# A fused attention and two-MLP kernel in float32: order of the chunks, sources and slots in the last product

## The chip, the cores and the metric

One core of a Trainium2 chip. The metric is the device time of one execution in microseconds (us), as the median of several runs. The engines are named as in the profile: PE (TensorE, matmuls), PEld (its weight loads), DVE (VectorE), ACT (ScalarE), POOL (GpSimd), SP (SyncE, which issues nearly all DMAs; "SPq" is its queue).

## The reference

Windowed attention over 4 batches of 8 heads, 576 positions, head size 64; then two MLPs over the 2304 tokens. Everything is float32.

```python
def _attn_ref(q, k, v):
    scores = scale * np.matmul(q, k.transpose(0, 1, 3, 2))
    mask = (rel >= 0) & (rel < 64)
    scores = np.where(mask, scores, -1000000000.0)
    ...                                  # softmax
    return np.matmul(attn, v)
def _moe_ref(x, w1, w2, w3, w_out):      # (2304,512) -> (2304,512)
    a = x @ w1
    b = x @ w2
    h = a * b @ w3
    return h @ w_out
def _moe2_ref(x, w_in, w_out):           # 512 -> 2048 -> 512
    h = x @ w_in
    g = np.maximum(0.01 * h, h)
    return g @ w_out
```

## The kernel before

**Splitting.** Each float32 operand of a large product is split into a high part (ACT, a Copy into float32r) and a low part (DVE, operand minus high part). A product is then three matmuls: high by high, high by low, low by high (`three_passes`, L367 to L369).

**Seven products.** Each large product is one level of a Strassen-like scheme: 7 products P1, P5, P6, P2, P7, P3, P4 (in this order) of half-size blocks. They share banks: P1, P6, P7 and P4 use one pair of banks (alpha), P5 and P3 another (gamma), P2 a third (beta). So copies and sums stand between them: ACT copies P1, P5 and P6 out (`copy_p1` L817, `copy_p5` L827, `copy_u2` L835), DVE adds P2, P7, P3 to these (`make_c11` L1237, `make_c22` L1247, `make_c12` L1257). In `bank_waits` P6 waits for the copy of P1, P7 for the copy of P6 (u2), P3 for the copy of P5, P4 for c22. Weight sums are made once (for w_out in rounds 2 to 9 by `out_sums`, stored in DRAM as `weight_sums`).

**Stages.** (1) w3 times moe w_out, 16 slots of pieces, beside the first attention steps. (2) 12 rounds of a and b and their product P, stored in DRAM as `p_between`. (3) The y product, 3 chunks of 768 tokens; 42 parts of P (`load_ty`, `split_ty` L848 and L1305) and then 7 blocks of x2. (4) The first product of the second MLP, 12 rounds r = HR0 to OR0 - 1, h = 0 to 11: four rounds for each of three chunks, a round making two of 16 row blocks of g for one chunk. Its 7 blocks of g (leaky ReLU on ACT L873 and L881, sums on DVE L1344, L1348, L1353) lie in `g_st` and are stored by SP as 7 DMAs of 384 KB into `g_between` (`store_g`, L570). (5) The second product: 84 parts k, in the order `T_SEQ` of (chunk, product, jp), jp = 0 to 3. A part is 2 x 768 columns of g from 384 KB: SP loads it (`load_t`, L587) into one of 8 slots `t_raw`, ACT and DVE split it (`split_t`, L897 and L1358) into block k modulo 7, PE does 12 matmuls of 384 columns on it (`second_product`). tk is part k's load.

**The slots.** `t_raw` 0 and 1 are spare places; 2 to 7 lie over `g_st` and can be used only when all of g is stored. So the first eight parts (`TEARLY`), all of chunk 0, go through slots 0 and 1 in turn; a load waits for the split of the part before it in its slot.

**The weights of the second product.** The 8 units of w_out (F_OUT to F_OUT + 7, here F0 to F7) take the place of the 8 units of w_in in the last four rounds (8 to 11), two per round: unit n is free when P4 has used it. SP loads a unit (L453 384 KB, L461 512 KB) into one of two places `unit_raw` when the split of the unit two before it is done; ACT (L767) and DVE (L1106) split it in two pieces each.

**Order.** All engines run lists written out in Python loops, in order; nothing is scheduled. An engine that waits holds everything behind it. In the old rounds 9 to 11 ACT does: copies of P1, split of the first late unit, copies of P5, (round 11: split t0), copies of u2, split of the second late unit, then the leaky steps.

## Time and profile before

| | us |
|---|---|
| median of 3 runs (all: 766.12, 770.91, 770.90) | 770.9 |
| the profiled execution | 769.24 |
| its span (first to last instruction) | 767.2 |
| PE busy | 747.2 |
| DVE busy | 531.9 |
| ACT busy | 420.6 |
| mean granted clock of PE | 0.991 |

The span is the time that the rows below cover; 2.0 us of the execution lie around it. "Granted clock" is the share of PE's full 2.4 GHz; a stretch at 0.50 is at 1.2 GHz. Times in rows are us from the start of the span. A matmul's row is longer than the step from one to the next, since they overlap.

### The profile page before, as it was taken

To read this page: it belongs to the slowest core of one execution; us is meant where nothing else is said; L and a number is where in the kernel's file an instruction comes from. 1 tells how busy PE (TensorE), PEld (TensorE's weight loads), DVE (VectorE), ACT (ScalarE), POOL (GpSimd) and SP (SyncE) were. 2 spreads that over 40 slices of the span, in tenths; PEclk is the share of its full clock that TensorE was granted. 3 is DMA by queue.
4 is the path that set the end of the run, shared out by engine and by line. 5 is a ranking of instruction groups with operands and counts; after the bars stand their busy time and mean duration, and the time that the engine had idled before them with its cause. 6 is when DMAs were issued, how large, how long until landed. Compare 5 with 4: busy or idle time off the path is not lost.

```text
span 767.2 us, 13105 instructions
## 1 busy us (share of the span) xinstructions
PE 747.2 (97%) x4744; PEld 720.9 (94%) x4744; DVE 531.9 (69%) x836; ACT 420.6 (55%) x901; POOL 95.3 (12%) x122
## 2 busy tenths in 40 slices
PE   8999999999999999999999999999897899999998
PEld 6787999999999999999999999999897799999998
DVE  4977998788656868698777968567786555455442
ACT  4866577546564344566646665454764544544441
POOL 1533374503243000000000000000000000000000
PEclk9999999999999999999999999999999899999999
DMA  9885777656873389889858888997997977778731
GB/s 327 283 288 165 233 231 235 216 156 214 283 226 129 127 268 343 298 247 331 296 192 296 305 304 304 327 306 246 400 370 241 385 209 238 211 205 231 218 108 62
DMA packets 100576, 192.89 MB, mean 251 GB/s; under 512 B 8224, under 2 KB 58272, under 8 KB 100512
## 3 DMA queue, kind: packets, MB, share of 16 engines
q1 hardware_dynamic: 94208, 179.08, 71.0%
q10 hardware_dynamic: 6304, 12.98, 4.4%
q8 instruction: 38, 0.62, 0.3%
q14 instruction: 26, 0.21, 0.1%
HBM read 120.06 MB, written 71.96 MB: 250 GB/s over the span
## 4 chain that ended last, share of the span: by engine, by line
PE 75%; DMA 9%; DVE 7%; ACT 3%; issue 3%; SPq 2%; POOL 1%; DVEq 0%; ACTq 0%
PE acc L367 13%; PE acc L369 13%; PE acc L368 13%; PE ps_scores L1565 3%; PE ps_more L367 3%; PE ps_more L369 3%; PE ps_more L368 3%; PE ps_values L1549 2%; PE ps_values L367 2%; PE ps_values L368 2%; PE ps_values L369 2%; PE ps_turned L1557 2%; PE ps_scores L367 2%; DMA p_between<-arena 2%; PE ps_scores L368 2%
## 5 line engine op out<-in xcount | busy, mean ns | idle before, releaser
L1358 DVE TENSOR_TENSOR parts<-arena,parts 128x768 fp32r<-128x768 f32 x72 | 68.5, 958 | 67.6 <-ACT parts L897 67.6
L367 PE MATMUL acc<-parts,weights_a 128*128 128x384 f32 (+1 forms) x300 | 105.8, 353 | 1.3 <-DVE arena L1295 0.7
L369 PE MATMUL acc<-parts,weights_a 128*128 128x384 f32 (+1 forms) x300 | 103.2, 344 | 0.0
L368 PE MATMUL acc<-parts,weights_a 128*128 128x384 f32 (+1 forms) x300 | 103.1, 344 | 0.0
L897 ACT ACTIVATE parts<-arena 128x768 fp32r<-128x768 f32 x72 | 60.6, 847 | 72.7 <-PE acc L369 35.0
L367 PE MATMUL acc<-parts,weights_b 128*128 128x384 f32 x296 | 99.9, 337 | 0.0
L369 PE MATMUL acc<-parts,weights_b 128*128 128x384 f32 x296 | 98.9, 334 | 0.0
L368 PE MATMUL acc<-parts,weights_b 128*128 128x384 f32 x296 | 98.9, 334 | 0.0
L778 ACT ACTIVATE arena<-arena,negmax 128x128 f32<-128x128 f32 x144 | 56.0, 391 | 28.4 <-DVE negmax L1144 28.4
L367 PEld LDWEIGHTS acc<-parts,weights_a 128*128 128x128 f32 x300 | 56.6, 189 | 5.3 <-DVE parts L1171 1.0
L369 PEld LDWEIGHTS acc<-parts,weights_a 128*128 128x128 f32 x300 | 56.5, 188 | 2.0
L368 PEld LDWEIGHTS acc<-parts,weights_a 128*128 128x128 f32 x300 | 56.7, 189 | 1.5
L873 ACT ACTIVATE arena<-arena 128x384 f32<-128x384 f32 x72 | 35.9, 525 | 40.5 <-DVE arena L1237 18.6
L367 PEld LDWEIGHTS acc<-parts,weights_b 128*128 128x128 f32 x296 | 55.6, 188 | 0.1
L368 PEld LDWEIGHTS acc<-parts,weights_b 128*128 128x128 f32 x296 | 55.6, 188 | 0.0
L369 PEld LDWEIGHTS acc<-parts,weights_b 128*128 128x128 f32 x296 | 55.6, 188 | 0.0
L848 ACT ACTIVATE parts<-arena 128x768 fp32r<-128x768 f32 x42 | 35.4, 848 | 33.7 <-PE ps_turned L369 10.7
L707 POOL TENSOR_TENSOR arena<-arena,rsum 128x512 f32<-128x512 f32 x36 | 37.5, 1042 | 126.1 <-DVE rsum L1152 126.1
L1305 DVE TENSOR_TENSOR parts<-arena,parts 128x768 fp32r<-128x768 f32 x42 | 39.6, 954 | 14.7 <-ACT parts L848 14.6
L1565 PE MATMUL ps_scores<-arena 128*128 128x128 f32 x288 | 38.1, 275 | 0.1
L1565 PEld LDWEIGHTS ps_scores<-arena 128*128 128x128 f32 x288 | 35.3, 192 | 0.6 <-issue 0.4
L1139 DVE SCALAR_TENSOR_TENSOR arena<-ps_scores,arena 128x512 f32<-128x512 f32 x36 | 24.6, 685 | 11.9 <-PE ps_scores L1565 11.5
(230 smaller groups left out, 1887.8 us busy)
## 6 DMA issues: line engine op xcount, KB each, us to landing
g_between<-arena SPq DMA_DIRECT2D x84, 384.0 KB, 4.8
arena<-g_between SPq DMA_DIRECT2D x84, 384.0 KB, 3.9
arena<-qk_steps SPq DMA_DIRECT2D x36, 512.0 KB, 4.2
arena<-p_between SPq DMA_DIRECT2D x42, 384.0 KB, 5.6
arena<-v_steps SPq DMA_DIRECT2D x36, 256.0 KB, 3.2
p_between<-arena SPq DMA_DIRECT2D x24, 384.0 KB, 5.2
x_between<-arena ACTq DMA_DIRECT2D x21, 384.0 KB, 5.2
arena<-x_between SPq DMA_DIRECT2D x21, 384.0 KB, 5.3
```

Of the source, the lines that this page charges most:

```text
L367: eng.matmul(out_ap, w_hi, m_hi, start=start, stop=False, skip_group_check=resumed)
L368: eng.matmul(out_ap, w_hi, m_lo, start=False, stop=False, skip_group_check=resumed)
L369: return eng.matmul(out_ap, w_lo, m_hi, start=False, stop=stop, skip_group_check=resumed)
L707: pool.tensor_tensor(probs[:, r], probs[:, r], rsum[:, r * HP:(r + 1) * HP].unsqueeze(2).to_broadcast([P, HP, KW]), ALU.mult).then_inc(pro ...
L778: act.activation(probs[:, r, u], probs[:, r, u], ACT.Exp, bias=negmax[:, r * HP + u:r * HP + u + 1], scale=1.0, accum_out=sums[:, r * HP + ...
L848: act.activation(block_places[k % NPROD][:, 0:BW], ty_raw[TY_SLOT[k]], ACT.Copy).then_inc(ty_hi, 1)
L873: act.activation(g, g, ACT.Prelu, alpha=SLOPE).then_inc(g_done[q], 1)
L897: act.activation(block_places[k % NPROD][:, 0:BW], t_raw[T_SLOT[k]], ACT.Copy).then_inc(t_hi, 1)
L1139: dve.scalar_tensor_tensor(out=probs[:, r], in0=ps_s[:, :].rearrange("p (h k) -> p h k", h=HP), scalar=float(D) ** -0.5, in1=picked.unsque ...
L1305: dve.tensor_tensor(b[:, BW:2 * BW], ty_raw[TY_SLOT[k]], b[:, 0:BW].bitcast(F32), ALU.subtract).then_inc(ty_lo, 1)
L1358: dve.tensor_tensor(b[:, BW:2 * BW], t_raw[T_SLOT[k]], b[:, 0:BW].bitcast(F32), ALU.subtract).then_inc(t_lo, 1)
L1565: last = pe.matmul(ps_s[:, w], qk[:, g % 2, w], qk[:, g % 2, DM + u * P:DM + (u + 1) * P], start=True, stop=True)
```

## The change

1. **Chunk order** `O_CHUNK = (2, 0, 1)`: the second product starts with the chunk made last. Its parts jp = 0 to 2 come from DRAM (rounds 8 to 10), its seven parts jp = 3 (round 11) are split from `g_st` itself (`T_HELD`, `t_source`, `t_ready`). Round 11 stores nothing, and 7 loads are left out. Inside products P6 to P4 of that chunk the held part comes first.
2. **Slots** are given out by `t_slots`: the place that was free first, slots 2 to 7 once the held blocks under them are split and the last sums are made.
3. **SP**: t0 and t1 are issued after round 10's last stores, not before its fills; t2 and t3 before F7; t4 and on after F7.
4. **Round 9**: F0 is split behind the copies of u2 (ACT) and c11 (DVE), F1 behind the leaky step of c22 (ACT) and c12 (DVE). Round 11's end: t3, F6, t4, F7.
5. **Parts of P**: 12 and 13 are issued in the last a and b round; 14 and 15 ahead of two fills.
6. **Start**: the mask and the pieces of slot 2 are loaded earlier, v(0), the first fill and v(1) later.

```diff
-TY_LOAD = {(9, 6): (0, 1), (10, 3): (2, 3), (10, 8): (4, 5), (11, 2): (6, 7), (11, 5): (8, 9)}
+TYEARLY = 10
+TY_LOAD = {..., (11, 5): (8, 9), (11, 9): (TYEARLY + 2,), (11, 11): (TYEARLY + 3,)}
...
-T_SLOT = [k % SPARE if k < TEARLY else (k - TEARLY + SPARE) % TRAW for k in range(TB)]
...
+O_CHUNK = (NC2 - 1, *range(NC2 - 1))
 T_SEQ = [(0, i, jp) for i, jp in ((0, 0), (0, 1), (0, 2), (1, 0), (1, 1), (1, 2), (0, 3), (1, 3))]
-T_SEQ += [(c, i, jp) for c in range(NC2) for i in range(NPROD) for jp in range(JP) if c > 0 or i > 1]
+T_SEQ += [(0, i, jp) for i in range(2, NPROD) for jp in (3, 0, 1, 2)]
+T_SEQ += [(c, i, jp) for c in range(1, NC2) for i in range(NPROD) for jp in range(JP)]
+T_HELD = [c == 0 and jp == JP - 1 for c, _, jp in T_SEQ]
+def t_slots():
+    freed = [-1, -1] + [1 + max(T_SEQ.index((0, i, JP - 1)) for i in pair) for pair in ((0, 1), (0, 1), (P6, P2), (P6, P2), (P7, P3), (P7, P3))]
+    ...
+        best = min(range(TRAW), key=lambda n: freed[n])
...
+        def t_source(k):
+            if T_HELD[k]:
+                return g_st[:, :, G_AT[T_SEQ[k][1]]]
+            return t_raw[T_SLOT[k]].rearrange("p (j t) -> p j t", j=2)
...
             def load_t(k):
-                c, i, jp = T_SEQ[k]
+                q, i, jp = T_SEQ[k]
+                if T_HELD[k]:
+                    return
+                c = O_CHUNK[q]
...
+                if T_SLOT[k] >= SPARE and T_USES[k] == 1:
+                    sp.wait_ge(gt2_made, 2 * HR)
+                    sp.wait_ge(gt4_made, 2 * HR)
+                if T_AFTER[k] > 0:
+                    sp.wait_ge(t_lo, T_AFTER[k])
...
+            sp.dma_start(mask_s[:, :], masks).then_inc(mask_in, 16)
             load_qk(1)
-            sp.dma_start(mask_s[:, :], masks).then_inc(mask_in, 16)
+            for i in pieces_for(2):
+                load_piece(i)
             load_v(0)
+            load_fill(0)
             load_v(1)
-            load_fill(0)
...
-                if h == HR - 2:
-                    for k in range(SPARE):
-                        load_t(k)
+                if h == HR - 1:
+                    load_t(0)
+                    load_t(1)
+                    load_fill(late)
+                    load_t(2)
+                    load_t(3)
+                    load_fill(late + 1)
+                    continue
...
-                if h > HR - ROUNDS:
+                if h > HR - ROUNDS + 1:
                     split_fill(late, 0)
                     split_fill(late, 1)
...
                 for s in range(2):
                     copy_u2(r, s)
...
+                if h == HR - ROUNDS + 1:
+                    split_fill(late, 0)
+                    split_fill(late, 1)
```

ScalarE in round 9, before: the copies of P1 (L817, banks ps_scores and ps_turned), the split of F0 (L767 into weights_a), the copies of P5 (L827) and of u2 (L835), the split of F1.

```order
L817 ACTIVATE arena<-ps_scores 128x384
L817 ACTIVATE arena<-ps_turned 128x384
L767 ACTIVATE weights_a<-arena 128x768
L767 ACTIVATE weights_a<-arena 128x1024
L827 ACTIVATE arena<-ps_values 128x384
L827 ACTIVATE arena<-ps_more 128x384
L835 ACTIVATE arena<-ps_scores 128x384
L835 ACTIVATE arena<-ps_turned 128x384
L767 ACTIVATE weights_a<-arena 128x768
L767 ACTIVATE weights_a<-arena 128x1024
L873 ACTIVATE arena<-arena 128x384 x6
```

The same place after (L860, L870, L878 are the copies, L810 the split of a unit, L916 the leaky step):

```order
L860 ACTIVATE arena<-ps_scores 128x384
L860 ACTIVATE arena<-ps_turned 128x384
L870 ACTIVATE arena<-ps_values 128x384
L870 ACTIVATE arena<-ps_more 128x384
L878 ACTIVATE arena<-ps_scores 128x384
L878 ACTIVATE arena<-ps_turned 128x384
L810 ACTIVATE weights_a<-arena 128x768
L810 ACTIVATE weights_a<-arena 128x1024
L916 ACTIVATE arena<-arena 128x384 x4
L810 ACTIVATE weights_a<-arena 128x768
L810 ACTIVATE weights_a<-arena 128x1024
```

F0's split has moved behind the copies of u2, F1's behind four of the six leaky steps.

SyncE's queue from the stores of round 9 to those of round 10, before: L570 stores g, L587 loads a part of g, L453 and L461 load a late unit.

```order
L570 DMA g_between<-arena 128x2x384 x6
L587 DMA arena<-g_between 128x768 x2
L453 DMA arena<-w_out_units 128x768
L461 DMA arena<-weight_sums 128x1024
L570 DMA g_between<-arena 128x2x384
L453 DMA arena<-w_out_units 128x768
L461 DMA arena<-weight_sums 128x1024
L570 DMA g_between<-arena 128x2x384 x6
```

After (L611 stores, L628 loads a part, L494 and L502 load a unit), on to the end of round 11:

```order
L611 DMA g_between<-arena 128x2x384 x6
L494 DMA arena<-w_out_units 128x768
L502 DMA arena<-weight_sums 128x1024
L611 DMA g_between<-arena 128x2x384
L494 DMA arena<-w_out_units 128x768
L502 DMA arena<-weight_sums 128x1024
L611 DMA g_between<-arena 128x2x384 x6
L628 DMA arena<-g_between 128x768 x2
L494 DMA arena<-w_out_units 128x768
L502 DMA arena<-weight_sums 128x1024
L628 DMA arena<-g_between 128x768 x2
```

The two loads of g that stood ahead of F4 now stand behind the six last stores of round 10; round 11's stores are gone.

ScalarE from the copies of P5 to those of u2 in round 11, after (L940 is the split of t0; before, the same rows with L827, L897 and L835):

```order
L870 ACTIVATE arena<-ps_values 128x384
L870 ACTIVATE arena<-ps_more 128x384
L940 ACTIVATE parts<-arena 128x768
L878 ACTIVATE arena<-ps_scores 128x384
L878 ACTIVATE arena<-ps_turned 128x384
```

Here nothing moved: the split of t0 keeps its place.

## Rows read from the trace of the kernel before

**Rows 1.** page: busy us by engine, and groups splitting g (busy, mean ns)
```profile
PE 747.2 (97%) x4744; PEld 720.9 (94%) x4744; DVE 531.9 (69%) x836; ACT 420.6 (55%) x901; POOL 95.3 (12%) x122
...
L1358 DVE TENSOR_TENSOR parts<-arena,parts 128x768 fp32r<-128x768 f32 x72 | 68.5, 958 | 67.6 <-ACT parts L897 67.6
...
L897 ACT ACTIVATE parts<-arena 128x768 fp32r<-128x768 f32 x72 | 60.6, 847 | 72.7 <-PE acc L369 35.0
```

**Rows 2.** waits of PE: total us, times, longest us
```profile
PE ps_values L367 <- DVE parts L1358: 4.1, 1, 4.1
PE acc L367 <- DVE weights_a L1358: 3.7, 1, 3.7
PE ps_scores L367 <- ACT arena L835: 3.5, 2, 2.2
```

**Rows 3.** timeline of PE: start, duration, instruction, [idle before <-releaser]
```profile
537.40 0.34 PE L369 MATMUL acc<-parts,weights_a 128*128 128x384 f32 x1
...
539.96 0.69 PE L367 MATMUL ps_scores<-parts,weights_a 128*128 128x384 f32 x1 [2.22 <-ACT arena L835]
...
543.22 0.33 PE L368 MATMUL ps_turned<-parts,weights_a 128*128 128x384 f32 x1
...
570.61 0.33 PE L367 MATMUL ps_scores<-parts,weights_b 128*128 128x384 f32 x1
...
582.92 0.34 PE L369 MATMUL acc<-parts,weights_b 128*128 128x384 f32 x1
...
599.17 0.69 PE L367 MATMUL acc<-weights_a,weights_b 128*128 128x384 f32 x1 [3.75 <-DVE weights_a L1358]
...
604.66 0.34 PE L369 MATMUL ps_more<-parts,weights_b 128*128 128x384 f32 x1
```

**Rows 4.** timeline of ACT, rounds 9 and 11
```profile
536.98 1.79 ACT L767 ACTIVATE weights_a<-arena 128x768 fp32r<-128x768 f32 x2 [4.96 <-DMA arena<-weight_sums]
...
539.42 0.49 ACT L835 ACTIVATE arena<-ps_scores 128x384 f32<-128x384 f32 x1
...
567.38 0.86 ACT L897 ACTIVATE parts<-arena 128x768 fp32r<-128x768 f32 x1
```

**Rows 5.** timelines of ACT and PE, start of the kernel
```profile
13.68 0.63 ACT L755 ACTIVATE parts<-arena 128x512 fp32r<-128x512 f32 x1 [4.39 <-DMA arena<-w_tiles]
...
15.77 0.50 PE L367 MATMUL acc<-parts 128*128 128x512 f32 x1 [1.79 <-DVE parts L1094]
```

**Rows 6.** timelines of ACT and PE, y product of chunk 0
```profile
324.00 0.85 ACT L848 ACTIVATE parts<-arena 128x768 fp32r<-128x768 f32 x1 [3.85 <-DMA arena<-p_between]
...
326.31 0.41 PE L367 MATMUL ps_scores<-parts,weights_b 128*128 128x384 f32 x1 [1.27 <-ACT arena L835]
```

**Rows 7.** stretch: us, busy by engine (PE first), PEclk, DMA share, GB/s
```profile
540.00:572.00 32.00, 32.00 (x177) 32.00 (x178) 26.14 (x41) 23.42 (x43) 0.00 (x0) 0.95 1.05 395
```

**Rows 8.** load of F2's second half (L461), issue and landing
```profile
L461 SPq DMA_DIRECT2D arena<-weight_sums x1: 760/760/760, 542.8 to 542.8; - x1
...
DMA to landing us min/median/max: 6.7/6.7/6.7
```

**Rows 9.** timelines of DVE and SP at the end of round 10
```profile
563.80 1.02 DVE L1353 TENSOR_TENSOR arena<-arena 128x384 f32<-128x384 f32 x2
...
568.03 0.75 SPq L453 DMA_DIRECT2D arena<-w_out_units  x1
```

**Rows 10.** landing of the load issued at 568.03 (L453)
```profile
DMA to landing us min/median/max: 5.5/5.5/5.5
```

**Rows 11.** landing of t0, issued at 553.55 (L587)
```profile
DMA to landing us min/median/max: 6.2/6.2/6.2
```

**Rows 12.** load t3 (L587), issue and landing
```profile
L587 SPq DMA_DIRECT2D arena<-g_between x1: 320/320/320, 575.2 to 575.2; - x1
...
DMA to landing us min/median/max: 3.7/3.7/3.7
```

**Rows 13.** landing of round 8's last two g stores (L570), 535 to 543
```profile
DMA to landing us min/median/max: 9.9/10.3/10.6
```

More of the change, by code:

```diff
@@ L153 @@
 TRAWY = 6
-TYEARLY = 10
 HRING = 4
@@ L182 @@
 T_SEQ = [(0, i, jp) for i, jp in ((0, 0), (0, 1), (0, 2), (1, 0), (1, 1), (1, 2), (0, 3), (1, 3))]
-T_SEQ += [(c, i, jp) for c in range(NC2) for i in range(NPROD) for jp in range(JP) if c > 0 or i > 1]
-T_USED = [sum(jp < JP - 1 for _, _, jp in T_SEQ[:k + 1]) for k in range(TB)]
+T_SEQ += [(0, i, jp) for i in range(2, NPROD) for jp in (3, 0, 1, 2)]
+T_SEQ += [(c, i, jp) for c in range(1, NC2) for i in range(NPROD) for jp in range(JP)]
+T_STEP = [sum(e[:2] == T_SEQ[k][:2] for e in T_SEQ[:k]) for k in range(TB)]
+T_USED = [sum(step < JP - 1 for step in T_STEP[:k + 1]) for k in range(TB)]
+T_HELD = [c == 0 and jp == JP - 1 for c, _, jp in T_SEQ]
+def t_slots():
+    freed = [-1, -1] + [1 + max(T_SEQ.index((0, i, JP - 1)) for i in pair) for pair in ((0, 1), (0, 1), (P6, P2), (P6, P2), (P7, P3), (P7, P3))]
+    uses, slot, after, count = [0] * TRAW, [], [], []
+    for k in range(TB):
+        best = min(range(TRAW), key=lambda n: freed[n])
+        if T_HELD[k]:
+            best = None
+        slot.append(best)
+        after.append(None if best is None else freed[best])
+        if best is not None:
+            uses[best] += 1
+            freed[best] = k + 1
+        count.append(None if best is None else uses[best])
+    return slot, after, count
+T_SLOT, T_AFTER, T_USES = t_slots()
 def build(nc, qk_steps, v_steps, masks, w3, wo, w12, w_in, w_out, out):
@@ L643, in _ @@
             load_ty(TYEARLY + 1)
+            load_ty(TYEARLY + 4)
+            load_ty(TYEARLY + 5)
             load_fill(F_IN + 2)
-            load_ty(TYEARLY + 2)
             load_fill(F_IN + 3)
-            for k in range(TYEARLY + 3, NTY):
+            for k in range(TYEARLY + 6, NTY):
                 load_ty(k)
@@ L1039, in _ @@
                 leaky(r, 2, c22_done)
+                if h == HR - ROUNDS + 1:
+                    split_fill(late + 1, 0)
+                    split_fill(late + 1, 1)
                 if last:
@@ L1050, in _ @@
                     leaky_c21(r, s)
-                    if h == HR - 1:
-                        split_fill(NFILL - 2 + s, 0)
-                        split_fill(NFILL - 2 + s, 1)
                 if last:
                     split_hx(NPROD * c + P7)
-            split_t(3)
-            for k in range(TROUND, TB + NPROD):
+            for n in range(2):
+                split_t(3 + n)
+                for part in range(2):
+                    split_fill(NFILL - 2 + n, part)
+            for k in range(TROUND + 1, TB + NPROD):
                 if k < TB:
@@ L1497, in _ @@
                     make_c12(r, s)
+                if h == HR - ROUNDS + 1:
+                    split_fill(late + 1, 0)
+                    split_fill(late + 1, 1)
                 if last:
@@ L1520, in _ @@
                     split_hx(NPROD * c + P7)
-            for k in range(TROUND, TB + NPROD):
+            for k in range(TROUND + 1, TB + NPROD):
                 if k < TB:
```

98 lines of the change are left out of this document (52 added, 46 removed).

## The prediction

> **What bounds the kernel now.** I read the busy shares, then what TensorE waits for, then the timelines around those waits, then the DMA landings. TensorE is busy 747.2 of 767.2 us [rows 1], so the change can win only where it idles or runs at half clock. Its waits are few [rows 2]: 4.1 and 3.7 us for splits of g (DVE L1358), 2.2 and 1.3 us for the copies of u2 (ACT L835). A matmul of 384 columns comes every 0.1734 us (71 steps from 570.61 to 582.92 [rows 3]), so 12 take 2.08 us and the 84 of a round 14.56.
>
> *Round 9.* Between the matmuls at 537.40 and 543.22 lie 11 steps, which should take 1.91 us and took 5.82 [rows 3]: 3.9 us lost, 2.4 of them the wait and 1.5 the half clock (1.2 GHz) that followed it. ScalarE stood 4.96 us before the split of the late weight unit F0 (F0 to F7: the units of w_out), whose DMA landed at 536.9, and the copies of p5 and u2 stood behind it [rows 4].
>
> *Into the second product.* From 582.92 to 604.66 there are 54 steps: 9.36 us of work in 21.74, 12.4 lost, and 0.1 more in the following steps: 12.5 us. Two waits and two stretches at half clock make them up; after the second, 17 steps took 5.49 us instead of 2.95, so 2.5 us went to the clock [rows 3].
>
> *Start and y product.* A wait of 1.79 us at 15.77 ends with a piece whose DMA ScalarE had awaited for 4.39 us, until 13.68 [rows 5]. A wait of 1.27 us at 326.31 has the same form: part 12 of P came from DRAM 3.85 us late and the copy of u2 stood behind it [rows 6]. Everything else is about 1.5 us of crumbs and is left alone.
>
> **Part 1, start.** Pieces 4 and 5 are issued before both loads of v, and before the two of the first fill. That is 1.0 MB less ahead of them, 2.6 us at the 395 GB/s of a full queue [rows 7]. The piece that came at 13.68 comes near 11, and the 1.8 us wait goes. Mask and qk change places at no cost: nothing waited for qk. VectorE paces this stretch in places, so I bound the gain by 0 and 2.1 us (the wait and a later 0.3) and take 1.8.
>
> **Part 2, parts 12 and 13 of P.** They are issued in the last round of a and b, behind parts 8 and 9, so they are there long before 320. Their slots need only splits 0 and 1. Gain 1.27 us and 0.24 of the slow first matmul (0.41 against 0.17): 1.5, at least 0.
>
> **Part 3, round 9.** F0 is split behind the copies of u2, F1 behind the leaky steps of c22. The copies then need no DMA, and product P7 starts at 537.57: 3.9 us back. But what comes next hangs on the DMA queue. It is full from 540 to 572 (share 1.05, 395 GB/s) [rows 7], so data lands when it did, while TensorE is 3.9 us earlier. F2 still lands at 542.8 + 6.7 = 549.5 [rows 8]; behind it ScalarE has its split, two copies of p5 and the first copy of u2, 2.9 us from start to end in round 9 (536.98 to 539.91 [rows 4]). So P7 of round 10 starts at 552.5, where it could at 552.1 (four products, 8.3 us, after 543.8): 0.4 us given back (0 to 2.5, the upper end with the half clock of rows 3). Net 3.5 us. The next neighbour, c22 of round 10 behind VectorE's split of F3, I find about 0.2 us ahead of P4; a miss there lies inside the same 2.5.
>
> **Part 4, the last chunk first.** Seven g stores and seven loads of g (2.7 MB each way) go. The first loads, t0 and t1, change place: before, SP issued t0 at 553.55, ahead of round 10's fills, and now behind the last store of round 10. Nothing is moved on ScalarE here: split t0 (L897) stays between the copies of p5 and of u2 of round 11 [rows 4]. So t0 is now a condition of P7 in round 11, which began at 570.61 [rows 3].
>
> When does t0 land? In the old trace round 10's last sum ended at 564.82 and the DMA behind the stores was issued at 568.03 [rows 9], 3.2 us later, and landed 5.5 us after that, at 573.5 [rows 10]. Now t0 stands in that place. Round 10's sums are some 2.5 us earlier (3.5 us, less 1 for DVE's wait for F3), which gives 565.5 for its issue. Two 384 KB loads less ahead of it give 2.0 us: 571.5. The other way, 565.5 plus 5.5 or 6.2 (the old t0 landed 6.2 after issue, also behind a burst of stores [rows 11]) gives 571.0 to 571.7. I take 571.5. Split 0.85 and the first copy of u2 0.5, with gaps, open P7 at 572.9. TensorE would be there at 570.6 - 3.5 = 567.1: a new wait of 5.8 us. The half clock behind it cost 1.5 to 2.5 us in rows 3; I take 2.0. Bounds: t0 lands 3.7 us after issue, as a load in a quiet queue did [rows 12], then P7 opens at 570.6 and this costs 3.5 + 1.5 = 5.0; or it lands 8 us after issue, then 7.8 + 2.5 = 10.3.
>
> From P7 on, first P7 to P4 (6.24 us) and 2.0: the second product starts at 572.9 + 8.2 = 581.1. Then the splits (0.85 on ScalarE, 0.96 on VectorE [rows 1]):
> - P7 at half clock ends near 576.8, its sums c22 at 577.5; behind them VectorE ends t1 at 578.3, and behind c12 t2 at 580.4.
> - t3's slot is free at 578.3; landed 3.7 later, 582.1; split on VectorE behind the g sums, 584.2. Part 3 is due at 587.3.
> - F6 and t4 are done at 587.2, part 4 is due at 589.4. F6 and F7 no longer queue with g stores.
> - t5 waits for t3's split, lands at 588.0 and is split behind F7 and the last g sums at 591.2; due at 591.5. This margin of 0.3 us is the thinnest.
> - parts 6, 7 and 8 come from where g lies, need no DMA, and let t9, t10, t11 run ahead.
>
> So the old 12.5 us go and 7.8 come: 4.7 us net (bounds 12.5 - 5.0 = 7.5, and 12.5 - 10.3 - 3 for waits at part 5 = -0.8). Later parts cost the same matmuls; chunks 0 and 1 were stored long before, and the last chunk's end is the same code.
>
> **Sum.** 1.8 + 1.5 + 3.5 + 4.7 = 11.5 us off the profiled execution's 769.24: 757.7. The runs' median is 770.9, their lowest 766.1, so the profiled one is 1.7 below the median and 3.1 above the lowest; between these I say 758.5.
>
> **Rivals.**
> - *t0 hides.* If the queue drains in round 10, or the splits arrive so that the copies of u2 run ahead of t0, the 7.8 us don't come: 751. For it: seven stores less, but those are round 11's, too late; against it: the queue's share of 1.05 and the order on ScalarE. Chance 0.13.
> - *t0 passes the stores.* It lands 3.7 us after issue, as in a quiet queue, and its wait costs 5.0 instead of 7.8: 755.7. The landings of 5.5 and 6.2 behind such bursts speak against it [rows 10, 11]. Chance 0.08. The Trainium skill, "DMA: Bandwidth & Descriptors", section "Queues, rings and completion order", would allow it: completion is not first in, first out per issuing engine, and a later DMA may finish its write before an earlier one.
> - *Splits too late at parts 3 to 5.* A landing 1.5 us longer than 3.7 adds 3 us at part 5 and another 1.5 of half clock: 763, and with a start that gains nothing, 765. Chance 0.17.
> - *The two-slot chain decides, slower.* t2 to t5 use only slots 0 and 1; t3 waits for t1's split and t5 for t3's. Every us of landing over 3.7 counts twice. With 10.6 us, the longest of the g stores of round 8 [rows 13], that is 13.8 - 0.3 + 2.5 = 16 us: 774. It passes the old time from landings of 8.1 us on. For it: such landings exist; against: they were seen in a full queue, and here only F7 is beside. Chance 0.05.
> - *The change does less than it says.* The held parts wait for the last leaky step and sums, and if DVE's new order (t3, F6, t4, F7, then the last sums) makes these late, the slots 2 and 3 open late and parts 11 on wait: 766. The held parts have 5 us of slack, so 0.05.
> - The forecast has 0.52, with its own range 755 to 763.
>
> A difference of 1%, 7.7 us, is about what a measurement tells from no change; the border is 763.2. The forecast and the first two rivals lie below it almost whole, the third half across, the fifth within 1%: faster 0.76, same 0.19, slower 0.05. The range reaches from the first rival to the third and fifth: 750 to 767.
>
> **What would show it.** Right: no wait for ACT L835's counterpart in round 9; a wait of about 5.8 us before P7 of round 11, released by the copy of u2, ScalarE idle before split t0 for a DMA out of g_between, and half clock behind it; no wait over 1 us in the second product; 1.8 and 1.3 us waits gone at the start and in the y product. Wrong: if P7 of round 11 doesn't wait, the queue was not the limit I take it for, and the time is near 751; if waits stand before parts 3 to 5, the landings in the new order are longer than 3.7 us; if the 1.8 us come back before 100 us, VectorE paces the start.

## The result, and the profile after

| | before | after |
|---|---|---|
| median, 4 runs of each on one chip (us) | 770.65 (766.12 to 770.91) | 760.14 (758.99 to 761.03) |
| profiled execution, its span | 769.24, 767.2 | 761.03, 759.2 |
| mean granted clock of PE | 0.991 | 0.996 |

The ratio is 0.9882, with a 95% interval of 0.9845 to 0.9919: about 9 us, or 6 to 12. The two medians lie 10.5 us apart, but one of the four runs of before is 4 us below the other three. Predicted were 758.5 us and 750 to 767. The time was right; the gain was less than the forecast's. Of its four terms one gave nothing that the times show, and another about 0.6 us on average.

Line numbers have moved: the copies of P1, p5 and u2 are now L860, L870 and L878, the split of a part is L940 (ACT) and L1410 (DVE), a load of g is L628, a store of g L611. The page's header and busy shares first, beside [rows 1]:

```profile
span 759.2 us, 13176 instructions
PE 743.8 (98%) x4744; PEld 717.4 (94%) x4744; DVE 530.9 (70%) x836; ACT 420.6 (55%) x901; POOL 96.1 (13%) x122
```

TensorE has the same 4744 matmuls and is busy 3.4 us less, mostly half clock that is gone; the other 4.6 of the 8.0 us of span are waiting. What TensorE waited for over the span (total, times, longest), beside [rows 2]:

```profile
PE ps_scores L387 <- ACT arena L878: 6.0, 1, 6.0
PE acc L387 <- DVE parts L1410: 1.5, 1, 1.5
PE ps_more L1791 <- POOL ident L744: 1.5, 1, 1.5
PE acc L387 <- DVE parts L1145: 1.2, 2, 0.9
PE acc L387 <- ACT arena L878: 0.6, 1, 0.6
```

The waits of 4.1, 3.7, 2.2 and 1.3 us are gone, and one of 6.0 and one of 1.5 (P6) stand in their place. The row of POOL is the wait for the first data of the kernel, at 1.52 us in both traces. The timeline of TensorE has three waits from round 10 on, beside [rows 3]:

```profile
549.73 0.44 PE L387 MATMUL acc<-parts,weights_b 128*128 128x384 f32 x1 [0.61 <-ACT arena L878]
...
570.74 0.69 PE L387 MATMUL ps_scores<-parts,weights_b 128*128 128x384 f32 x1 [5.99 <-ACT arena L878]
...
597.92 0.41 PE L387 MATMUL acc<-parts,weights_b 128*128 128x384 f32 x1 [1.49 <-DVE parts L1410]
```

They are P7 of round 10, P7 of round 11, and the first matmul of P6 in the second product (part 8). ScalarE at the second and third of these places, beside [rows 4]:

```profile
561.49 0.48 ACT L870 ACTIVATE arena<-ps_more 128x384 f32<-128x384 f32 x1
569.46 0.84 ACT L940 ACTIVATE parts<-arena 128x768 fp32r<-128x768 f32 x1 [7.49 <-DMA arena<-g_between]
570.21 0.47 ACT L878 ACTIVATE arena<-ps_scores 128x384 f32<-128x384 f32 x1
...
592.79 0.85 ACT L940 ACTIVATE parts<-arena 128x768 fp32r<-128x768 f32 x1 [2.54 <-DMA arena<-g_between]
595.09 1.58 ACT L940 ACTIVATE parts<-arena 128x768 fp32r<-128x768 f32 x2 [1.45 <-DMA arena<-g_between]
596.58 0.82 ACT L940 ACTIVATE weights_a<-arena 128x768 fp32r<-128x768 f32 x1
597.31 0.85 ACT L860 ACTIVATE arena<-acc 128x384 f32<-128x384 f32 x2
```

The first three rows are the predicted wait as it was predicted: ScalarE stands 7.5 us before the split of t0, the copy of u2 is behind it, and TensorE starts P7 0.06 us after the end of that copy. In the last four, the copy of P1 stands behind the splits of parts 10 to 13, and P6 needs the bank that this copy empties; the experiments take that up, since the profile names VectorE for this wait. The landing of t0, issued at 563.09 behind round 10's last stores, beside [rows 11]:

```profile
DMA to landing us min/median/max: 6.3/6.3/6.3
```

And the stretches (busy by engine with PE first, granted clock, DMA share, GB/s), beside [rows 7]:

```profile
560.00:565.00 5.00, 4.75 (x28) 4.43 (x26) 2.24 (x3) 1.97 (x4) 0.00 (x0) 1.00 1.05 387
565.00:570.00 5.00, 0.00 (x0) 0.00 (x0) 0.00 (x0) 0.54 (x1) 0.00 (x0) 0.94 0.99 333
570.00:575.00 5.00, 4.26 (x13) 4.26 (x14) 4.37 (x7) 4.57 (x9) 0.00 (x0) 0.50 0.44 151
575.00:580.00 5.00, 5.00 (x27) 5.00 (x27) 4.22 (x6) 3.15 (x7) 0.00 (x0) 0.87 0.51 153
```

In such a row the first figure is the length of the stretch, the next five are the busy times, and the seventh is the granted clock. TensorE runs 13 matmuls in the third stretch, where full clock has room for 25: half clock (1.2 GHz) from 570.7 to 576.3, 17 steps in 5.58 us where 2.95 would do, so 2.6 us behind a wait of 6.0.

At the start and in the y product, beside [rows 5, 6], the row of 1.79 us is gone, a smaller one has come 5 us earlier, and ScalarE has no wait for a DMA near 324:

```profile
10.69 0.50 PE L387 MATMUL acc<-parts,weights_a 128*128 128x512 f32 x1 [0.90 <-DVE parts L1145]
```

### The profile page after: what moved, and what is told of

It reads as the page before. It is cut to its first block, busy times and chain, and to the rows that moved or that the text cites. A ratio compares the mean times of both kernels' runs of the same rounds, so it can differ in the third digit from the quotient of the medians.

```text
span 759.2 us, 13176 instructions
## 1 busy us (share of the span) xinstructions
PE 743.8 (98%) x4744; PEld 717.4 (94%) x4744; DVE 530.9 (70%) x836; ACT 420.6 (55%) x901; POOL 96.1 (13%) x122
## 4 chain that ended last, share of the span: by engine, by line
PE 75%; DMA 9%; DVE 7%; issue 3%; ACT 3%; SPq 2%; POOL 1%; DVEq 0%; ACTq 0%
PE acc L387 13%; PE acc L389 13%; PE acc L388 13%; PE ps_scores L1623 3%; PE ps_more L387 3%; PE ps_more L389 3%; PE ps_more L388 3%; DMA g_between<-arena 3%; PE ps_values L1607 2%; PE ps_turned L1615 2%; PE ps_values L387 2%; PE ps_values L388 2%; PE ps_values L389 2%; PE ps_scores L387 2%; PE ps_turned L389 2%
## 5 line engine op out<-in xcount | busy, mean ns | idle before, releaser
L1410 DVE TENSOR_TENSOR parts<-arena,parts 128x768 fp32r<-128x768 f32 x72 | 68.7, 957 | 71.7 <-ACT parts L940 71.7
L940 ACT ACTIVATE parts<-arena 128x768 fp32r<-128x768 f32 x72 | 60.7, 847 | 77.9 <-PE acc L389 35.0
L916 ACT ACTIVATE arena<-arena 128x384 f32<-128x384 f32 x72 | 35.8, 525 | 40.3 <-DVE arena L1288 18.5
```

The costliest lines, as they stand in the source:

```text
L916: act.activation(g, g, ACT.Prelu, alpha=SLOPE).then_inc(g_done[q], 1)
L940: act.activation(block_places[k % NPROD][:, 0:BW].rearrange("p (j t) -> p j t", j=2), t_source(k), ACT.Copy).then_inc(t_hi, 1)
L1410: dve.tensor_tensor(lo, t_source(k), hi.bitcast(F32), ALU.subtract).then_inc(t_lo, 1)
```

## Three intervals that all runs are read by

TensorE's instructions are the same in every kernel here, so the same matmul can be found in each trace, and the time between two of them compared. Three intervals, from the starts of the rows of TensorE's timeline: (s) the start of the 49th matmul of 512 columns, which tells what the start has cost so far; (y) from the 1,009th to the 1,401st matmul of 384 columns, the first part of the y product; (z) from the 2,251st to the 3,501st, which is from round 8 nearly to the end. Without waits and at full clock, z would be 1250 x 0.1734 = 216.8 us.

| kernel | s | y | z | ratio to before, 95% |
|---|---|---|---|---|
| before | 25.38 | 69.46 | 233.33 | |
| before_round9 | 25.89 | 67.95 | 232.06 | 0.9995 [0.9985, 1.0006] |
| after | 23.39 | 67.95 | 228.52 | 0.9882 [0.9845, 0.9919] |
| after_again | 22.45 | 67.95 | 228.01 | 0.9897 [0.9877, 0.9916] |
| after_round9_back | 23.30 | 67.95 | 227.54 | 0.9897 [0.9877, 0.9916] |
| after_y_back | 23.09 | 68.14 | 227.39 | 0.9886 [0.9868, 0.9904] |
| after_start_back | 24.90 | 67.94 | 228.71 | 0.9936 [0.9914, 0.9958] |
| order_alone | 26.22 | 68.70 | 228.23 | 0.9931 [0.9915, 0.9947] |
| split_behind_u2 | 23.18 | 67.95 | 225.33 | 0.9871 [0.9853, 0.9888] |
| t0_in_round10 | 22.71 | 67.95 | 225.96 | 0.9876 [0.9858, 0.9895] |
| copy_p1_early | 22.71 | 67.95 | 226.19 | 0.9860 [0.9841, 0.9879] |
| t0_r10_copy_early | 22.70 | 67.95 | 223.29 | 0.9824 [0.9808, 0.9840] |
| sums_later | 22.99 | 67.94 | 220.18 | 0.9788 [0.9772, 0.9804] |
| sums_later_round9_back | 22.66 | 67.94 | 219.53 | 0.9783 [0.9765, 0.9801] |

From the 2,651st to the 3,501st matmul all of them take 147.33 or 147.34 us. Whatever the kernels differ by in z happens before it.

The ratios are against runs of the kernel before on the same chip. The intervals of the ratios are 0.8 to 2.8 us to either side, so differences between two kernels of under 2 us are read from z as much as from the time.

## Experiments

**after_again**: the changed kernel once more, as the measure for the three others of its group.

> The changed kernel once more, as the measure for the three kernels beside it. Both theories: 760 us, within 1 us of its four runs (758.99 to 761.03), with a wait of 6 us before P7 of round 11.

Measured: 759.45 us (757.76 to 760.74), before beside it 767.4. The wait before P7 of round 11 is 5.2 us in this trace. The gain is 7.9 us by this ratio, 9.1 by the first; the kernel before had medians of 767.4, 768.1 and 768.7 us in the three later groups of runs (13, 9 and 11), not the 770.9 of its first three.

**before_round9**: the new order of round 9 alone, put into the kernel before. The three places below in ScalarE's list are behind the copies of P1, of u2, and behind the leaky step of c22; VectorE's list changes in the same way.

```diff
-                if h > HR - ROUNDS:
+                if h > HR - ROUNDS + 1:
                     split_fill(late, 0)
                     split_fill(late, 1)
 ...
-                if h > HR - ROUNDS:
+                if h == HR - ROUNDS + 1:
+                    split_fill(late, 0)
+                    split_fill(late, 1)
+                if h > HR - ROUNDS + 1:
                     split_fill(late + 1, 0)
                     split_fill(late + 1, 1)
 ...
                 leaky(r, 2, c22_done)
+                if h == HR - ROUNDS + 1:
+                    split_fill(late + 1, 0)
+                    split_fill(late + 1, 1)
```

> The kernel before with one part of the change alone: in round 9 F0 is split behind the copies of u2 and F1 behind the leaky step of c22 (ACT) and c12 (DVE). Theory A (the stall of 3.9 us goes, and the full DMA queue takes some back, since F2 lands when it did): no wait before P7 of round 9, one of 0.4 to 0.8 us before P7 of round 10, and from round 11 on the loads in slots 0 and 1, which hang on the queue and on splits, keep the waits of 4.1 and 3.7 us or lengthen them a little: 767 us at the profile, 2 to 3 us less than the kernel before beside it. Theory B (all 3.9 us are kept): 3.9 us less. Theory C (the queue gives nothing back to TensorE): the waits into the second product grow by the whole 3.9 us: no difference.

Measured: 767.0 us, ratio 0.9995 [0.9985, 1.0006]. By the time it is theory C: nothing. The wait in round 9 is gone and TensorE is ahead at the 2,401st matmul by 3.2 us more than at the 2,251st, as the forecast said. But the waits of TensorE in this trace are

```profile
PE ps_values L367 <- DVE parts L1364: 5.3, 1, 5.3
PE acc L367 <- DVE weights_a L1364: 3.4, 1, 3.4
```

5.3 us where before waited 4.1, for the same part 3. At the 2,601st matmul 1.4 of the 3.2 us are left, and 1.3 in z. So the waits for the splits of g take back more than half in this trace, not all as theory C has it, and the times show nothing of what is left.

**split_behind_u2**: the split of t0 stands behind the copies of u2 and the leaky steps of c11 (ACT), behind c22 (DVE). If the wait of 6.0 us is the order on ScalarE, it goes.

```diff
-                if h == HR - 1:
-                    split_t(0)
                 for s in range(2):
                     copy_u2(r, s)
 ...
                 if h == HR - 1:
+                    split_t(0)
                     split_t(1)
```

The diff shows ScalarE's list; the same is done in VectorE's.

> The changed kernel, with the split of t0 moved behind the copies of u2 and the first leaky step of round 11 on ACT, and behind c22 on DVE; the loads keep their place. Theory A (the split's place in ACT's queue makes the wait of 6.2 us before P7 and the 2.6 us of half clock behind it): no wait before P7 of round 11. The second product could then start near 570.5 instead of 579.6; t0, landed at 569.4, is split at 571.3, and t2 to t5, which go through two slots, hold parts 2 to 5: waits of 1 to 2 us each, part 6 some 3 to 4 us earlier than now. 756 to 757 us. Theory B (the landings set the end whatever the order): the waits before parts 0 to 5 add up to what the wait before P7 was, 760 us.

**t0_in_round10**: t0 and t1 are loaded in round 10, behind its fill F4 and its second store of g, so that they land before ScalarE comes to them.

```diff
                 if h == HR - 1:
-                    load_t(0)
-                    load_t(1)
                     load_fill(late)
 ...
                 if h > HR - ROUNDS:
                     load_fill(late)
+                if h == HR - 2:
+                    load_t(0)
                 store_g(r, 0)
 ...
                 store_g(r, 1)
+                if h == HR - 2:
+                    load_t(1)
```

> The changed kernel, with the load of t0 issued in round 10 right behind F4's, and that of t1 behind round 10's second store of g; all splits keep their place. Theory A (the place of t0 in the DMA queue makes the wait): t0 lands near 561, the wait before P7 of round 11 is under 1 us; t2 lands 2 us later than the stores of round 10, near 573.5, and holds part 2 by some 1.5 us, t4 and t5 hold theirs by as much: 756 us. Theory B (the queue is full, so each transfer only trades places with another): F5 or the stores come 2 us later, and the waits before the second product's parts 2 to 5 give all back: 760 us.

Measured: split_behind_u2 757.59 us, ratio 0.9871 [0.9853, 0.9888]; t0_in_round10 757.84 us, ratio 0.9876 [0.9858, 0.9895]. These intervals overlap with those of the changed kernel, so what follows is read from z. In both the wait of 6.0 us and the half clock behind it, 8.6 us together, are gone; from the 2,251st to the 2,501st matmul TensorE is 8 to 9 us faster. Yet z is shorter by only 2.1 to 3.2 us. That is more than theory B's nothing and under theory A's 3 to 4 us. The rest has gone into waits that did not exist. TensorE in t0_in_round10:

```profile
578.82 0.45 PE L387 MATMUL ps_values<-parts,weights_a 128*128 128x384 f32 x1 [1.42 <-DVE parts L1412]
...
581.70 0.44 PE L387 MATMUL ps_values<-parts,weights_a 128*128 128x384 f32 x1 [0.52 <-DVE parts L1412]
...
585.51 0.44 PE L387 MATMUL ps_values<-parts,weights_b 128*128 128x384 f32 x1 [1.43 <-DVE parts L1412]
...
593.92 0.41 PE L387 MATMUL acc<-parts,weights_b 128*128 128x384 f32 x1 [1.87 <-DVE parts L1412]
```

These are parts 3, 4 and 5, and P6. split_behind_u2 has the same four, of 1.42, 0.49, 1.45 and 1.80 us, and 0.5 us before part 2. The wait for t0 was in front of a chain of splits that was hardly earlier than TensorE. Both ways of taking it out give the same time, so what is behind it sets the gain, and not how it was removed.

**copy_p1_early**: which wait is the one at 597.92 in the changed kernel? ScalarE copies P1 right behind the split of part 10.

```diff
             for k in range(TROUND + 1, TB + NPROD):
                 if k < TB:
                     split_t(k)
+                if k == NPROD + 3:
+                    for s in range(2):
+                        copy_p1(OR0, s)
 ...
-                        if i == P1:
+                        if i == P1 and c > 0:
```

> Edit: in the changed kernel ScalarE copies P1 of the second product's first chunk right behind the split of part 10, no longer behind those of parts 11, 12 and 13. Theory A (the 1.5 us wait before P6's first matmul in the changed kernel, which the profile puts down to VectorE's split, is in truth the wait for the copy of P1, which stood behind splits whose DMAs landed late): the wait goes, 757.9 us beside 759.5 for the changed kernel. Theory B (the profile's name is right, the split of part 8 is late): the wait stays and the time is 759.5.

Measured: 757.63 us, ratio 0.9860 [0.9841, 0.9879]. Theory A. The wait has left the list of waits, z is 1.8 to 2.3 us shorter than in the two traces of the changed kernel, and ScalarE now does

```profile
591.44 0.85 ACT L940 ACTIVATE parts<-arena 128x768 fp32r<-128x768 f32 x1 [2.88 <-DMA arena<-g_between]
592.37 1.01 ACT L860 ACTIVATE arena<-acc 128x384 f32<-128x384 f32 x2
593.75 1.59 ACT L940 ACTIVATE parts<-arena 128x768 fp32r<-128x768 f32 x2 [0.36 <-DMA arena<-g_between]
```

The copy comes before the split of part 11, whose DMA ScalarE would otherwise have waited for. The profile's name for the wait, DVE L1410, was that of another condition of the same matmul; the last thing it waited for was ScalarE's copy at 597.31.

**t0_r10_copy_early**: both.

> Edit: load of t0 behind the fill F4's and t1's behind the second g store of round 10, as in t0_in_round10, and the copy of P1 early, as in copy_p1_early. Theory A (both are places where TensorE waits, one behind the other, so they add): 757.8 less 1.5 to 1.9 and less the half clock behind it, 755.5 us. Theory B (whatever is won before P6 is waited for again at P6 or later, for parts 11 to 16): 757.5 us, with a wait of 1.5 us or more before a later part.

Measured: 754.97 us, ratio 0.9824 [0.9808, 0.9840]. Theory A, they add: z is 223.29, 2.7 less than with t0 early alone and 2.9 less than with the copy early alone. Waits of 1.42, 0.49 and 1.44 us are left before parts 3, 4 and 5. VectorE in that stretch:

```profile
573.90 0.96 DVE L1415 TENSOR_TENSOR parts<-arena,parts 128x768 fp32r<-128x768 f32 x1 [4.28 <-ACT parts L942]
574.78 0.95 DVE L1400 TENSOR_TENSOR arena<-arena 128x768 f32<-128x768 f32 x1
575.76 0.56 DVE L1404 TENSOR_TENSOR arena<-arena 128x384 f32<-128x384 f32 x1
576.24 0.95 DVE L1400 TENSOR_TENSOR arena<-arena 128x768 f32<-128x768 f32 x1
577.23 0.56 DVE L1404 TENSOR_TENSOR arena<-arena 128x384 f32<-128x384 f32 x1
577.70 0.95 DVE L1415 TENSOR_TENSOR parts<-arena,parts 128x768 fp32r<-128x768 f32 x1
578.57 2.09 DVE L1162 TENSOR_TENSOR weights_b<-arena,weights_b 128x768 fp32r<-128x768 f32 x2
```

VectorE has no idle time from 573.90 on (12.03 of the 13 us to 586 are busy). The split of t3 starts at 577.70 behind four sums of g; TensorE gets part 3 at 578.71. The sums are for the held parts 7 and 8; part 7 starts at 589.7, 12 us later.

**sums_later**: the same, with the second pair of sums behind the split of part 6 and the last sums behind that of part 8.

```diff
                 g_sums13(r, 0)
                 g_sum2(r, 0)
-                g_sums13(r, 1)
-                g_sum2(r, 1)
-                if h == HR - 1:
+                if h < HR - 1:
+                    g_sums13(r, 1)
+                    g_sum2(r, 1)
+                else:
                     split_t(3)
 ...
+                    split_t(5)
+                    split_t(6)
+                    g_sums13(r, 1)
+                    g_sum2(r, 1)
 ...
+                if k == NPROD + 1:
+                    for s in range(2):
+                        g_sum4(OR0 - 1, s)
```

> Edit: t0_r10_copy_early, and on VectorE the second pair of sums of g of round 11 (2 operations, 1.5 us) stands behind the split of part 6 and no longer ahead of that of part 3, the last sums (1.0 us) behind that of part 8 and no longer ahead of that of part 5. Theory A (with t0 early, the three waits of 1.4, 0.5 and 1.4 us before parts 3, 4 and 5 come from VectorE's queue, which is busy 11.4 of the 12 us from 578 to 590): 1.5 to 2.5 us less than t0_r10_copy_early, near 753.5. Theory B (the landings of t3, t4 and t5 set them, through the two slots they share): the same time as t0_r10_copy_early, with ScalarE waiting for DMAs ahead of the splits by as much as the sums gave.

Measured: 752.13 us, ratio 0.9788 [0.9772, 0.9804]. Theory A, and more than its 1.5 to 2.5: z is 3.1 us shorter than in t0_r10_copy_early. This kernel beats both the one before and the changed one, by 16 us and by 7 to 8. From round 10 on TensorE waits in it only for

```profile
574.10 0.44 PE L387 MATMUL acc<-parts,weights_b 128*128 128x384 f32 x1 [0.55 <-DVE parts L1415]
...
579.39 0.45 PE L387 MATMUL ps_values<-parts,weights_a 128*128 128x384 f32 x1 [0.58 <-DVE parts L1415]
...
582.26 0.44 PE L387 MATMUL ps_values<-parts,weights_b 128*128 128x384 f32 x1 [0.51 <-DVE parts L1415]
```

and 0.20 us in round 10.

**after_round9_back**: the changed kernel with round 9 as before. The diff is before_round9's turned round.

> Edit: the changed kernel with round 9's splits of F0 and F1 where they were before (F0 ahead of the copies of p5 and u2, F1 ahead of the leaky steps). In the kernel before, the new order alone gave nothing (ratio 0.9995). Theory A (the forecast's: it is worth 3.5 us, which the wait for t0 doesn't swallow): 763 us. Theory B (P7 of round 11 waits for t0, which comes from a DMA queue that is full from 540 us on, so TensorE's lead of 3.2 us at round 10 only lengthens that wait): within 1 us of the changed kernel, 760, with the wait before P7 of round 11 near 3 us instead of 6.0.

Measured: 759.94 us, ratio 0.9897 [0.9877, 0.9916], the same ratio as after_again. Theory B. TensorE waits 1.95 us at P7 of round 9 and 0.65 at P4, and then

```profile
570.91 0.69 PE L387 MATMUL ps_scores<-parts,weights_b 128*128 128x384 f32 x1 [4.09 <-ACT arena L878]
```

P7 of round 11 starts at 570.91 after a wait of 4.09, where the changed kernel started it at 570.74 after 5.99. Theory B had a wait near 3. Counted from the 2,251st matmul, TensorE came 2.1 us later than in the changed kernel and went on only 0.2 us later. The half clock behind the wait then cost 1.4 us here and 2.6 in the changed kernel, which leaves this one 1.0 us ahead in z.

**sums_later_round9_back**: is round 9 worth something when that wait is gone?

> Edit: sums_later (t0 early, copy of P1 early, sums of g later) with round 9's splits of F0 and F1 back where they were before. Theory A (round 9's new order was worth nothing only because TensorE then waited for t0; with that wait gone it is worth the 2 to 3 us lost at P7 of round 9): 754 to 755 us beside 752.1 for sums_later. Theory B (the full DMA queue up to the 572nd us and the splits of t3 to t5 behind it set when the second product goes on, whatever TensorE's lead): 752.1 to 752.7.

Measured: 751.7 us, ratio 0.9783 [0.9765, 0.9801]. Theory B again, even here. The waits of 1.3 and 0.7 us in round 9 are back, and the three before parts 2, 4 and 5 are gone instead. The reason stands on SyncE and ScalarE. First sums_later, the loads of t2 and t3 and the split of t2:

```profile
568.68 0.80 SPq L628 DMA_DIRECT2D arena<-g_between  x2
...
572.21 0.85 ACT L942 ACTIVATE parts<-arena 128x768 fp32r<-128x768 f32 x1 [4.97 <-DMA arena<-g_between]
```

and the same two in sums_later_round9_back:

```profile
568.74 1.97 SPq L628 DMA_DIRECT2D arena<-g_between  x2
...
572.22 0.85 ACT L942 ACTIVATE parts<-arena 128x768 fp32r<-128x768 f32 x1 [2.16 <-DMA arena<-g_between]
```

t2 holds what round 10 stored, so its load waits for those stores to land. SyncE's waits say so, 5.8 us in sums_later and 3.9 in the other:

```profile
SPq L620 <- DMA g_between<-arena: 5.8, 1, 5.8
```

```profile
SPq L620 <- DMA g_between<-arena: 3.9, 1, 3.9
```

The five stores are issued from 557.3 on in the one and from 559.2 on in the other, and the last lands at 568.5 and 568.6. From 540 to 565 the queue is full in both, with a DMA share of 1.04 and 1.05:

```profile
540.00:565.00 25.00, 24.80 (x143) 24.48 (x142) 22.76 (x32) 19.76 (x36) 0.00 (x0) 1.00 1.04 397
```

```profile
540.00:565.00 25.00, 24.32 (x141) 24.26 (x141) 20.16 (x31) 18.41 (x34) 0.00 (x0) 1.00 1.05 406
```

Since the two traces do not reach round 8 at the same time, the better measure is the time from the 2,251st matmul. The last store of round 10, issued and landed (us), in the three pairs of kernels that differ in round 9 alone:

| pair | old order | new order |
|---|---|---|
| before, before_round9 | 40.6, 46.9 | 39.1, 47.0 |
| after_round9_back, after | 40.0, 45.4 | 39.0, 45.8 |
| sums_later_round9_back, sums_later | 39.3, 46.2 | 38.1, 46.9 |

With the new order the store is issued 1.0 to 1.5 us earlier and lands 0.1 to 0.7 us later. So while this queue is full, it ends no earlier for stores that join it earlier. Why it ends a little later I have not shown.

**after_start_back**: the changed kernel with the loads of the start as before.

```diff
+            load_qk(1)
             sp.dma_start(mask_s[:, :], masks).then_inc(mask_in, 16)
-            load_qk(1)
-            for i in pieces_for(2):
-                load_piece(i)
             load_v(0)
+            load_v(1)
             load_fill(0)
-            load_v(1)
             for k in range(WSLOTS):
-                for i in pieces_for(k + 2) if k else ():
+                for i in pieces_for(k + 2):
                     load_piece(i)
```

> Edit: the changed kernel with the loads of the start in the order of before (mask behind qk of step 1, both v and the first fill ahead of the pieces of slot 2). Theory A (the start is worth its whole lead of 2.0 us, since TensorE is busy without a wait from the 25th us to the 300th): 761.5 us beside 759.5 for the changed kernel, and the wait of 1.8 us near the 15th us is back. Theory B (the time won is taken back where TensorE waits for a DMA or the DMA queue paces, in the transitions at 320, 550 and 565): 759.5 to 760.

Measured: 763.18 us (761.17 to 765.43), ratio 0.9936 [0.9914, 0.9958]. Theory A, and more: 0.0039 to 0.0054 above the changed kernel, 3 to 4 us by the time. By s it is less: the ten profiles with the new start have 22.45 to 23.39, mean 22.92, the four with the old one 24.90 to 26.22, mean 25.60, so 2.7 us. The wait is back (1.68 us at 15.30). Of the four with the old start, the two without half clock behind this wait (24.90 and 25.38) are 2.2 us above the new start's mean, the two with it (25.89 and 26.22) 3.1. The lead is still there at round 8: the 2,251st matmul stands at 522.2 us in the nine profiles with the new start and the new order of P, and at 524.5 in the four with the old start, less what y lost in them: 2.3 us. The profile of after_start_back itself shows only 0.8 of it there; it is of one of the two fastest of its executions (761.51 us).

**after_y_back**: the changed kernel with parts 12 to 15 of P loaded as before.

```diff
-TY_LOAD = {..., (11, 5): (8, 9), (11, 9): (TYEARLY + 2,), (11, 11): (TYEARLY + 3,)}
+TY_LOAD = {..., (11, 5): (8, 9)}
 ...
-            load_ty(TYEARLY + 4)
-            load_ty(TYEARLY + 5)
             load_fill(F_IN + 2)
+            load_ty(TYEARLY + 2)
             load_fill(F_IN + 3)
-            for k in range(TYEARLY + 6, NTY):
+            for k in range(TYEARLY + 3, NTY):
                 load_ty(k)
```

> Edit: the changed kernel with the loads of parts 12 and 13 of P issued as before, behind the stores of the last round of a and b, and the fills between them as before. Theory A (the forecast's, from the profile of before with its wait of 1.27 us): 761.0 us, 1.5 more than the changed kernel. Theory B (that wait differs from execution to execution: the profile of before_round9, with the same code there, shows no wait over 0.3 us before the copy of u2 in the y product and ScalarE waiting 1.7 us for the DMA, where before waited 3.85): 759.5 to 760, within 0.7 us of the changed kernel.

Measured: 759.87 us, ratio 0.9886 [0.9868, 0.9904], against 0.9882 and 0.9897 for the changed kernel. That is theory B; by the times alone a loss of 1.5 us could still hide in the intervals, so y decides. ScalarE waits for the DMA,

```profile
321.36 0.85 ACT L890 ACTIVATE parts<-arena 128x768 fp32r<-128x768 f32 x1 [2.44 <-DMA arena<-p_between]
```

but TensorE does not: no wait of it between 300 and 340 us is over 0.15. Four profiles have the old order here, with y of 69.46, 67.95, 68.14 and 68.70: 1.5 us lost in one, 0.0, 0.2 and 0.8 in the others. The ten with the new order all have 67.94 or 67.95. So the edit takes away a wait that comes in some executions, some 0.6 us on average by these four.

**order_alone**: start, P and round 9 all as before, so that only the chunk order, the held parts and the slots are left.

> Edit: the changed kernel with start, parts of P and round 9 all as before, so that only the last chunk first, its held parts and the slots are left of the change. Theory A (the forecast's prices: 1.8 for the start, 1.5 for P, 3.5 for round 9, 4.7 for the chunk order): 759.5 + 6.8 = 766.3 us, a gain of 1.9 over before at most. Theory B (round 9 is worth nothing, since the wait for t0 swallows it, as after_round9_back showed; start 2.0, P 0 to 1.5): 761.5 to 763, so the chunk order holds more than half of the change's gain.

Measured: 763.41 us (761.58 to 764.29), ratio 0.9931 [0.9915, 0.9947], and z of 228.23. The time is 0.4 us above theory B's range and 2.9 below theory A's 766.3. The new chunk order alone is worth 5.3 us by the ratio (0.0069 x 768.7, interval 4.1 to 6.5) and 5.1 by z (233.33 - 228.23). Its t0:

```profile
572.83 0.84 ACT L937 ACTIVATE parts<-arena 128x768 fp32r<-128x768 f32 x1 [5.74 <-DMA arena<-g_between]
```

Counted from the 2,251st matmul, the split of t0 starts 46.6 us later here, 47.0 in after_round9_back, 46.8 and 46.7 in the two traces of the changed kernel. So an earlier TensorE in round 9 does not bring it forward. A lead won before round 8 does: that matmul stands at 526.2 us here and between 521.5 and 523.2 in the other traces with t0 behind the stores, and in all eight t0 lands 46.1 to 46.9 us after it.

## Why the prediction was right, and where not

The sum by its terms, forecast and measured (us):

| term | forecast | measured |
|---|---|---|
| Part 1, start | 1.8 | 2.7 (mean of s), 3 to 4 (time) |
| Part 2, parts 12 and 13 of P | 1.5 | 0.6 (mean of y); the times show none of it |
| Part 3, round 9 | 3.5 | 0 (time), in three pairs of kernels |
| Part 4, chunk order | 4.7 | 5.1 to 5.3, without round 9's lead |
| Parts 3 and 4 together | 8.2 | 4.8 and 5.3 (z, two traces) |
| sum | 11.5 | 8 to 9 |

*Why the time still came out.* In part this was luck. The forecast took its 11.5 us off a base of 770.0, between a median of 770.9 and a profiled execution of 769.24; the kernel before has medians of 767.4 to 768.7 in its later runs. A gain too large by 2.4 to 3.6 us was taken off a base too high by 1.3 to 2.6. The terms also made up for each other in part: the start gave more than its price, parts 2 and 3 less. And the range of 17 us would have held the result with part 3 at nothing.

*Part 1* was mis-sized, above its own bound of 2.1. That bound was the wait and a crumb. It left out half clock behind the wait, which the trace of before did not have and those of order_alone and before_round9 do (below), and this adds some 1.5 us to an execution with the old start.

*Part 2* was priced from one execution. The wait of 1.27 us in [rows 6] was the longest in four executions of that order. The bound "at least 0" was the right one to stand near.

*Part 3* is the step that failed as a price: "Net 3.5 us". The step itself happened: no wait in round 9, and 0.61 us at P7 of round 10 where 0.4 were forecast. What failed is that it was added up. The same paragraph said that the queue is full and "data lands when it did", and used this for F2. Part 4 then dropped it: it let round 10's sums, the issue of t0 and its landing move forward "some 2.5 us" with TensorE, which kept the 3.5 us alive. after_round9_back shows the contrary: t0's split 46.7 to 47.0 us after the same matmul with either order. The lead of 2.1 us made the wait for t0 1.9 us longer, 5.99 for 4.09, and there was 1.2 us more of half clock behind it. Three pairs of kernels (before_round9, after_round9_back, sums_later_round9_back) put the worth of round 9 at no more than about 2 us either way, and the first of them at under 1.2.

*Part 4* named the new wait, its place, its releaser and its size: 5.8 + 2.0 us, measured 6.0 + 2.6. The size of the wait came out because two errors went the same way: with the 2,251st matmul put where before has it, TensorE came to P7 at 567.9 (forecast 567.1) and P7 opened at 573.9 (forecast 572.9). In the six other traces with this wait the half clock behind it cost 1.4 to 2.9 us. The rival in which t0 passes the stores fell with the landing of 6.3 us; t0 landed 0.9 us after the last store. By the Trainium skill, "DMA: Bandwidth & Descriptors", section "Queues, rings and completion order", completion is not first in, first out per issuing engine; the rule allows such a passing, and no run here shows it for these loads. The waits at parts 3 to 5 did not come, and the margins were as forecast: their splits ended 2.9, 2.1 and 0.4 us before TensorE needed them (forecast 3.1, 2.2 and 0.3). In t0_in_round10, where TensorE comes to these parts 6 to 8 us earlier, the same parts waited 3.4 us. What the forecast did not see is P6: it checked the held parts 6 to 8 for their data and not for the bank, and the copy of P1 that empties it stood behind the splits of three later parts that wait for DMAs. That was 1.5 us, and copy_p1_early takes it out.

*The net of the whole transition.* Before to after, z fell by 4.8 us in this trace and by 5.3 in after_again; forecast for parts 3 and 4 together were 8.2. Of the 3.4 us that are missing in the first, P7 of round 11 opening later than forecast is 1.0, the half clock behind it 0.6, and the wait at P6 1.5. So the path through the changed kernel was forecast to within 1 us up to P7. What was wrong is the price of round 9's share in it, and P6 was not seen.

What stays open: the start is worth 2.3 to 2.7 us by the profiles and 3 to 4 by the times, whose interval reaches down to about 1. I have not separated the edits within it, the mask, the pieces and v.

## What to carry to other kernels

For a lead that an engine wins while the DMA queue is full, ask whether the queue ends earlier by it. If what follows waits for data behind that queue, the lead becomes a longer wait of about the same size, as round 9's did here, while the lead won at the start, before the queue filled, moved the whole of it. And where a long wait is taken out, look first at the engine that feeds the next five steps: here VectorE had no idle time left, and 2.5 us of sums that were due much later stood ahead of splits that TensorE was waiting for.

## What the hardware showed that I had not expected

*The same wait with and without half clock.* In before, a wait of 1.79 us at 15.77 had full clock behind it; in order_alone one of 1.80 us at 15.67, at the same matmul, had half clock. The code of the start is the same in four kernels: before and after_start_back (1.68 us) kept full clock, order_alone and before_round9 (1.82 us) did not. The stretch from 10 to 20 us in before, then in order_alone (the seventh figure is PEclk):

```profile
10.00:20.00 10.00, 8.21 (x46) 6.83 (x44) 6.14 (x11) 5.57 (x21) 2.89 (x4) 1.00 1.03 389
```

```profile
10.00:20.00 10.00, 8.20 (x32) 6.61 (x33) 6.21 (x10) 5.66 (x21) 2.99 (x4) 0.83 1.01 384
```

In order_alone the matmuls of 512 columns come every 0.43 us from 16.5 to 19.5, where before has every 0.23; the twelve steps behind the wait take 4.45 us for 2.90, so 1.5 us more are lost. In the second product a wait of 1.80 us had full clock behind it in split_behind_u2, and one of 1.87 at the same matmul in t0_in_round10 half clock (1.2 GHz): steps of 0.32 us for 0.17 from 594.7 to 597.9, 1.5 us again. So in this kernel a wait under 2 us cost nothing more, or 1.5 us more, and a bound should hold both.

*The tail of a full queue.* The last store of round 10 was issued 1.9 us apart in sums_later and sums_later_round9_back and landed within 0.06 us, at 568.5 and 568.6. Counted from the 2,251st matmul, it was issued 1.2 us earlier in sums_later and landed 0.7 us later.
